# Attention and two expert layers on one core: three tiles' keys and queries fetched as 32x32 squares, one DMA per norm

## The reference, cut to what matters

```python
keep = is_sink | in_window
scores = np.where(keep, scale * q @ k.T, -1e9)
a = np.exp(scores - scores.max(-1, keepdims=True))
attn = (a / (a.sum(-1, keepdims=True) + 1e-9)) @ v      # per batch and head
x = attn.transpose(0, 2, 1, 3).reshape(1536, 512)
x = sum(p[:, e:e+1] * (np.maximum(x @ w1[e], 0) @ w2[e]) for e in range(4))
h = x @ w_in
out = (h * np.cos(h)) @ w_out
```

## Time and profile before

| | us |
|---|---|
| median of 3 runs | 834.82 |
| lowest, highest | 834.08, 837.19 |
| the profiled execution | 837.64 |
| its span | 835.9 |
| TensorE busy in the span | 831.0 (99%) |
| VectorE, ScalarE, GpSimd busy | 455.7, 458.0, 551.7 |
| DMA queue of SyncE | 28.5% of 16 engines |

### The profile page before, as it was taken

The page is one execution under the profiler, slowest core; times in us unless marked ns, Lnnn a source line. Parts: engine busy times, 40 slices in busy tenths (PEclk is TensorE's granted clock), DMA queues, the critical chain, the costliest instruction groups (busy, mean ns, idle before and its releaser), DMA issues.

```text
span 835.9 us, 13778 instructions
## 1 busy us (share of the span) xinstructions
PE 831.0 (99%) x4564; PEld 743.6 (89%) x4564; DVE 455.7 (55%) x947; ACT 458.0 (55%) x985; POOL 551.7 (66%) x417
## 2 busy tenths in 40 slices
PE   9999999999999999999999999999999999999998
PEld 7777989988988988988988998998998998998997
DVE  4988833523523427633433433338767749756756
ACT  5888734334334435433423523525867869867864
POOL 3777996476476778575475575878384399685450
PEclk9999999999999999999999999999999999999999
DMA  8785231211221220432331131130223430530202
GB/s 184 169 190 147 67 123 51 102 61 44 98 68 44 91 83 19 117 105 53 95 112 50 52 101 51 51 101 30 73 63 76 125 117 0 177 102 18 84 1 76
DMA packets 101045, 70.46 MB, mean 84 GB/s; under 512 B 68368, under 2 KB 74864, under 8 KB 100976
## 3 DMA queue, kind: packets, MB, share of 16 engines
q1 hardware_dynamic: 100976, 69.58, 28.5%
HBM read 62.96 MB, written 3.19 MB: 79 GB/s over the span
## 4 chain that ended last, share of the span: by engine, by line
PE 96%; DVE 1%; issue 1%; ACT 1%; DMA 0%; SPq 0%; ACTq 0%; DVEq 0%
PE scores L1499 11%; PE scores L1503 11%; PE scores L1501 11%; PE scores L1512 10%; PE scores L1514 10%; PE scores L1510 10%; PE bank L1512 5%; PE bank L1514 5%; PE bank L1510 5%; PE bank L1499 3%; PE bank L1501 3%; PE bank L1503 3%; PE scores L1406 2%; PE bank L1441 2%; PE bank L1417 1%
## 5 line engine op out<-in xcount | busy, mean ns | idle before, releaser
L665 POOL TENSOR_TENSOR w_lo<-w_raw,w_hi 128x512 fp32r<-128x512 f32 x96 | 129.8, 1362 | 139.0 <-ACT w_hi L814 139.0
L1499 PE MATMUL scores<-x_hi,w_hi 128*128 128x384 f32 x528 | 177.1, 335 | 0.4 <-DVE x_lo L1136 0.2
L1503 PE MATMUL scores<-x_hi,w_lo 128*128 128x384 f32 x528 | 176.8, 335 | 0.0
L1501 PE MATMUL scores<-x_lo,w_hi 128*128 128x384 f32 x528 | 176.5, 334 | 0.0
L672 POOL TENSOR_TENSOR w_lo<-w_raw,w_hi 128x1024 fp32r<-128x1024 f32 x48 | 116.2, 2431 | 65.4 <-ACT w_hi L824 65.4
L824 ACT ACTIVATE w_hi<-w_raw 128x1024 fp32r<-128x1024 f32 x48 | 50.9, 1060 | 190.2 <-PE scores L1514 188.8
L1514 PE MATMUL scores<-w_hi,h_lo 128*128 128x512 f32 x384 | 149.3, 389 | 0.0
L1512 PE MATMUL scores<-w_lo,h_hi 128*128 128x512 f32 x384 | 149.3, 389 | 0.0
L1510 PE MATMUL scores<-w_hi,h_hi 128*128 128x512 f32 x384 | 149.0, 388 | 0.0
L1240 DVE SCALAR_TENSOR_TENSOR acc<-scores,probs,acc 128x512 f32<-128x512 f32 x56 | 41.8, 749 | 116.5 <-PE scores L1514 116.5
L1499 PEld LDWEIGHTS scores<-x_hi,w_hi 128*128 128x128 f32 x528 | 99.1, 188 | 2.4 <-issue 0.7
(11 more groups left out here) (140 smaller groups left out, 1548.0 us busy)
## 6 DMA issues: line engine op xcount, KB each, us to landing
w_raw<-in_moe_w_dram SPq DMA_DIRECT2D x30, 1024.0 KB, 5.1
w_raw<-in_moe_w_in_dram SPq DMA_DIRECT2D x8, 1024.0 KB, 5.0
w_raw<-in_moe_w_out_dram SPq DMA_DIRECT2D x8, 1024.0 KB, 5.4
v_nat<-in_v_dram SPq DMA_DIRECT2D x12, 256.0 KB, 4.0
norm<-routing_dram SPq DMA_DIRECT2D x24, 128.0 KB, 3.2
x_t<-t_sum SPq DMA_DIRECT2D x192, 16.0 KB, 1.9
k_nat<-in_k_dram SPq DMA_DIRECT2D x11, 256.0 KB, 3.8
q_nat<-in_q_dram SPq DMA_DIRECT2D x11, 256.0 KB, 3.6
```

Of the source, the lines that this page charges most:

```text
L665: nc.gpsimd.tensor_tensor(w1_slots(w1_lo, h % 2, part), w1_part(h % 2, part), w1_slots(w1_hi, h % 2, part).bitcast(F32), ALU.subtract)\
L1499: nc.tensor.matmul(target[:, 0:HALF], w1_hi[:, i, slot, d], x_hi[:, n - 1, d], start=first and d == 0, stop=False, skip_group_check=True)
L1501: nc.tensor.matmul(target[:, 0:HALF], w1_hi[:, i, slot, d], x_lo[:, n - 1, d], start=False, stop=False, skip_group_check=True)
L1503: last = nc.tensor.matmul(target[:, 0:HALF], w1_lo[:, i, slot, d], x_hi[:, n - 1, d], start=False, stop=d == 1, skip_group_check=True)
```

## The change

Four things. (1) For the tiles 9, 10 and 11 (SQUARED = 9) there are no loads into `k_nat` and `q_nat` and no transposes by TensorE. 16 DMAs fetch the keys of all three, 16 the queries: each takes one head's 32 columns at 384 positions, 48 KB in pieces of 128 bytes, and places them in 32 partitions, so that a 32x32 transpose of each square by VectorE (`nc.vector.transpose`) gives the tile of `k_t` or `q_t` straight from SBUF. SyncE issues them at the end of its loop's steps t = 2 to 7: 4, 6, 6 for the keys, 6, 6, 4 for the queries. (2) Query copies: tiles 1, 7 and 8 by VectorE, 2 to 6 by ScalarE, 9 to 11 by the new transposes. (3) `load_norm` is one DMA instead of two. The sums stand in another order (even heads first), so that its source is 2 rows of 512 numbers, each read 64 times, and its target 128 partitions of 2 KB. (4) The first two of the first batch's token sums go from VectorE (rounds 18 and 20) to GpSimd (rounds 17 and 19).

```diff
-QUERIES_BY_DVE = (7, 8, 9)
+QUERIES_BY_DVE = (1, 7, 8)
+    SQUARED = T - 3
+    SQUARE_PARTS = 2 * H
+        q_squares = sb("q_squares", [P, PAIRS, HALF], stack=early)
+        k_squares = x_t[:, 1, :, HALF:S]
+        def sum_at(h):
+            return h % 2 * PAIRS + h // 2
...
-            return routing[at:at + rows, :].rearrange("(p r s) e -> p r (s e)", p=PAIRS, r=2)
+            return routing[at:at + rows, :].rearrange("(h s) e -> h (s e)", h=H)
...
+            def load_squares(dst, src, first, last, signal):
+                for n in range(first, last):
+                    h, f = divmod(n, 2)
+                    p, r = divmod(h, 2)
+                    rows = slice((2 * r + f) * 32, (2 * r + f + 1) * 32)
+                    source = src[1, h, (SQUARED - TPB) * P:S, f * 32:(f + 1) * 32]
+                    sp.dma_start(dst[rows, p, :].rearrange("j (c i) -> j c i", i=32),
+                                 source.rearrange("(c j) i -> j c i", j=32)).then_inc(signal, 16)
...
             def load_norm(t):
                 sp.wait_ge(inverse_stored[t % 2], 16 * (t // 2 + 1))
                 if t >= 2:
                     sp.wait_ge(x_ready, t - 1)
-                for r in range(2):
-                    sp.dma_start(norm[r * D:(r + 1) * D, t % 2],
-                                 sums_in_memory(t)[:, r].unsqueeze(0).broadcast_to([D, PAIRS, P]))\
-                        .then_inc(norm_landed[t % 2], 16)
+                sums = sums_in_memory(t).rearrange("(r p) s -> r (p s)", r=2)
+                sp.dma_start(norm[:, t % 2].rearrange("p k s -> p (k s)"),
+                             sums.unsqueeze(1).broadcast_to([2, D, PAIRS * P])).then_inc(norm_landed[t % 2], 16)
...
-                if 5 <= t + 3 < T:
+                if 5 <= t + 3 < SQUARED:
                     load_keys(t + 3)
...
+                if t == 2:
+                    load_squares(k_squares, k, 0, 4, k_squares_landed)
...
+                elif t == 7:
+                    load_squares(q_squares, q, 12, 16, q_squares_landed)
...
@@ GpSimd's rounds
+                if i in (17, 19):
+                    sum_tokens(0, (17, 19).index(i))
@@ VectorE
+                    n = t - SQUARED
+                    nc.vector.transpose(target, k_squares[:, :, n * P:(n + 1) * P]).then_inc(k_ready, 1)
...
+            def turn_queries(t):
+                dve.wait_ge(q_squares_landed, 16 * SQUARE_PARTS)
+                dve.wait_ge(scores_done, PAIRS * (t - 1))
+                n = t - SQUARED
+                nc.vector.transpose(q_t[:, t % 2], q_squares[:, :, n * P:(n + 1) * P]).then_inc(q_squares_ready, 1)
...
-                if i in (18, 20, 21, 23):
-                    sum_tokens((18, 20, 21, 23).index(i))
+                if i == 21:
+                    sum_tokens(2)
+                elif i == 23:
+                    sum_tokens(3)
@@ TensorE's rounds
-                if i % 2 == 1 and (i + 3) // 2 < T:
+                if i % 2 == 1 and (i + 3) // 2 < SQUARED:
                     turn_keys((i + 3) // 2)
-                elif i >= 2 and i % 2 == 0 and i // 2 + 1 < T:
+                elif i >= 2 and i % 2 == 0 and i // 2 + 1 < SQUARED:
                     turn_queries(i // 2 + 1)
```

More of the change, by code:

```diff
@@ L110, in program @@
         x_hi = sb("x_hi", [P, 7, 2, HALF], F32R)
+        early = ExitStack()
+        sb("early_lo", [P, 2, 2, HALF], stack=early)
+        q_squares = sb("q_squares", [P, PAIRS, HALF], stack=early)
+        early.close()
         x_lo = sb("x_lo", [P, 7, 2, HALF], F32R)
@@ L186, in program @@
         first_landed = [sem("first_keys_landed"), sem("first_queries_landed")]
+        k_squares_landed = sem("k_squares_landed")
+        q_squares_landed = sem("q_squares_landed")
         probs_landed = sem("probs_landed")
@@ L204, in program @@
         q_ready = sem("q_ready")
+        q_squares_ready = sem("q_squares_ready")
         k_sink_kept = sem("k_sink_kept")
@@ L427, in store_inverse @@
                 sp.wait_ge(inverse_copied, t + 1)
-                sp.dma_start(sums_in_memory(t).rearrange("p r s -> (p r) s"), inverse[sum_rows(t), t % 2, :])\
+                sp.dma_start(sums_in_memory(t), inverse[sum_rows(t), t % 2, :])\
                     .then_inc(inverse_stored[t % 2], 16)
@@ L518, in _ @@
                     load_values(t)
+                if t == 2:
+                    load_squares(k_squares, k, 0, 4, k_squares_landed)
+                elif t == 3:
+                    load_squares(k_squares, k, 4, 10, k_squares_landed)
+                elif t == 4:
+                    load_squares(k_squares, k, 10, 16, k_squares_landed)
+                elif t == 5:
+                    load_squares(q_squares, q, 0, 6, q_squares_landed)
+                elif t == 6:
+                    load_squares(q_squares, q, 6, 12, q_squares_landed)
+                elif t == 7:
+                    load_squares(q_squares, q, 12, 16, q_squares_landed)
                 if t == TPB + 1:
@@ L647, in normalise @@
                 pool.wait_ge(x_copied, t + 1)
-                pool.wait_ge(norm_landed[t % 2], 32 * (t // 2 + 1))
+                pool.wait_ge(norm_landed[t % 2], 16 * (t // 2 + 1))
                 g, i = divmod(t, TPB)
@@ L780, in exp_head @@
                                      bias=neg_max[:, t, h:h + 1], scale=-1.0,
-                                     accum_out=row_sum[:, t, h:h + 1]).then_inc(exp_ready, 1)
+                                     accum_out=row_sum[:, t, sum_at(h):sum_at(h) + 1]).then_inc(exp_ready, 1)
             def copy_own(d):
@@ L792, in copy_queries @@
                 act.wait_ge(q_turned, t + 1)
[L793 to L796, removed]
+                act.wait_ge(scores_done, PAIRS * (t - 1))
+                nc.scalar.activation(q_t[:, t % 2], turn_bank[:].rearrange("p (k s) -> p k s", k=PAIRS), ACT.Copy)\
                     .then_inc(q_ready, 1)
@@ L916, in _ @@
                     exp_head(i, 1)
-                if i == 1:
-                    copy_queries(1)
                 if 0 <= i - TURN_LAG < ND:
@@ L923, in _ @@
                     exp_head(i, 3)
-                if i >= 2 and i % 2 == 0 and i // 2 + 1 < T and i // 2 + 1 not in QUERIES_BY_DVE:
+                if i >= 2 and i % 2 == 0 and i // 2 + 1 < SQUARED and i // 2 + 1 not in QUERIES_BY_DVE:
                     copy_queries(i // 2 + 1)
@@ L1063, in copy_keys @@
             def copy_keys(t):
-                dve.wait_ge(k_turned, t + 1)
+                if t < SQUARED:
+                    dve.wait_ge(k_turned, t + 1)
+                else:
+                    dve.wait_ge(k_squares_landed, 16 * SQUARE_PARTS)
                 if t >= 3:
@@ L1068, in copy_keys @@
                     dve.wait_ge(k_sink_kept, (t - 3) // TPB + 1)
-                nc.vector.tensor_copy(k_t[:, :, t % 3, 0:P], turn_bank[:].rearrange("p (k s) -> p k s", k=PAIRS))\
-                    .then_inc(k_ready, 1)
+                target = k_t[:, :, t % 3, 0:P]
+                if t < SQUARED:
+                    nc.vector.tensor_copy(target, turn_bank[:].rearrange("p (k s) -> p k s", k=PAIRS))\
+                        .then_inc(k_ready, 1)
+                else:
+                    n = t - SQUARED
+                    nc.vector.transpose(target, k_squares[:, :, n * P:(n + 1) * P]).then_inc(k_ready, 1)
             def copy_queries(t):
                 dve.wait_ge(q_turned, t + 1)
+                if t >= 2:
+                    dve.wait_ge(scores_done, PAIRS * (t - 1))
+                source = out_bank if t == 1 else turn_bank
+                nc.vector.tensor_copy(q_t[:, t % 2], source[:].rearrange("p (k s) -> p k s", k=PAIRS))\
+                    .then_inc(q_ready, 1)
+            def turn_queries(t):
+                dve.wait_ge(q_squares_landed, 16 * SQUARE_PARTS)
                 dve.wait_ge(scores_done, PAIRS * (t - 1))
-                nc.vector.tensor_copy(q_t[:, t % 2], turn_bank[:].rearrange("p (k s) -> p k s", k=PAIRS))\
-                    .then_inc(q_ready, 1)
+                n = t - SQUARED
+                nc.vector.transpose(q_t[:, t % 2], q_squares[:, :, n * P:(n + 1) * P]).then_inc(q_squares_ready, 1)
             def copy_sinks(t):
@@ L1123, in sum_tokens @@
             def sum_tokens(n):
[L1125 to L1128, removed]
+                dve.wait_ge(x_summed, n)
                 nc.vector.tensor_tensor(*token_sum(0, n)).then_inc(x_summed, 1)
@@ L1150, in _ @@
                     copy_keys(1)
+                if i == 1:
+                    copy_queries(1)
                 if i % 2 == 1 and (i + 3) // 2 < T:
                     copy_keys((i + 3) // 2)
-                elif i % 2 == 0 and i // 2 + 1 in QUERIES_BY_DVE:
+                elif i >= 2 and i % 2 == 0 and i // 2 + 1 in QUERIES_BY_DVE:
                     copy_queries(i // 2 + 1)
+                elif i % 2 == 0 and SQUARED <= i // 2 + 1 < T:
+                    turn_queries(i // 2 + 1)
                 if i % 2 == 0 and 0 <= (i - 2) // 2 < T:
@@ L1390, in scores @@
```

(5 more changed lines are left out.)

## The result

The changed kernel takes 859.21 us (median of 5 runs, 858.72 to 860.08), the kernel before 834.82. The ratio is 1.0291, with a 95% interval of 1.0274 to 1.0308. The forecast was 857, slower.

What follows compares the result with a forecast made beforehand. TensorE was taken to set the attention stage's pace; after the change, two DMA engines carrying every norm would, with 70.6 us of work ending the stage 21.7 us later: +22 us, 857 us, likely 850 to 866, wider range 832 to 868.

Steps and rivals of the forecast that it cites:

- Where the norm runs: Norm DMA: with 2 outermost in its source, each norm runs on the same two engines, 128 KB apiece.
- The price of a norm: Norm DMA on two engines: 5.6 us of work taken, bounds 3.8 to 8.9; landing 7.7 us after issue.
- 2.1 + 5.6: Norm's issue to landing: 2.1 us fixed plus 5.6 us for 128 KB on each of two engines.
- The sum: Two engines' work from norm 0 to norm 7: 70.6 us, values of round 23 at 104.5, +22 us overall.
- the terms: Work on the two engines: 5.6 us per norm, 1.12 per 256 KB load, 0.35 per square, 1.4 for w2.
- the two parts of w2 (1.4): DMA engines: two 256 KB parts of the w2 weights, 1.4 us together in the two engines' work.
- GpSimd's sums and VectorE's moves: Sums of 1.85 us each cost nothing to 1.5 us; VectorE's moves, about 0.69 us each, near zero.
- SyncE's queue: SyncE's issuing: squares at 0.6 us each delay norms up to 3 us, costing GpSimd between nothing and 3 us.
- that case: Rival where norms land like before or sooner: 2.6 us saved, 0 to 2.5 taken back, 832 to 835 us.
- the forecast's own case: Attention stage: the norm's two engines become the pace, 857 us, range 850 to 866, chance 0.74.

Runs made afterwards that it cites:

- experiment 1: The changed kernel with the norm in two DMAs again, 64 repeats outermost, pieces still 2 KB: 840.40 us, ratio 1.0053.
- experiment 2: The kernel before with only the norm's single DMA, sums in the new order: 851.81 us, ratio 1.0193.
- experiment 4: The changed kernel with the norm as two DMAs of half the columns, each with 2 rows outermost: 867.78 us, ratio 1.0390.
- experiment 3: The changed kernel with the store of the next tile's sums issued ahead of the norm instead of behind it: 861.12 us, ratio 1.0307.
- experiment 5: The changed kernel with two norm DMAs and the two token sums back on VectorE: 841.32 us, ratio 1.0077.
- experiment 6: The kernel before with only the two token sums moved to GpSimd: 836.15 us, ratio 1.0014.
- experiment 8: The kernel before with only the last three tiles' keys as squares, 16 DMAs spread 3, 3, 3, 3, 4 over steps 2 to 6: 834.29 us, ratio 0.9991.
- experiment 9: The kernel before with only 16 key squares, packed 4, 6, 6 in steps 2 to 4: 840.63 us, ratio 1.0061.
- experiment 7: The kernel before with sums in the new order, its two norm DMAs reading 2 KB pieces: 834.03 us, ratio 0.9990.

## Why the prediction was right, point by point

*Where the norm runs.* Right. That the source's outermost count of 2 puts the norm on two engines was read from a count of packets; experiments 1, 2 and 4 bear it out each in its way, and the signals fit to the unit in the changed kernel and in all three. What the Trainium skill adds ("DMA: Bandwidth & Descriptors", the section on why a DMA increments its semaphore by 16), that it is always the lowest-numbered engines, agrees with experiment 4 as far as that can show it: two DMAs in a row share their pair. Which engines those are no run here shows.

*The price of a norm.* Right. A norm issued at 26.80 was used at 34.59, one issued at 92.67 at 100.69: 7.8 and 8.0 us, where 2.1 + 5.6 were taken. All eight lie between 7.2 and 8.0, 7.7 on the mean.

*The sum.* Right, and by its own terms, for most of the way. The norms of the changed kernel left at 26.80, 37.74, 48.38, 59.64, 68.36, 76.83, 84.84 and 92.67. In steps 3 to 5 (a norm, three loads, six squares) the terms give 5.6 + 3.4 + 2.1 = 11.1 us; the gaps are 10.9, 10.6 and 11.3. In step 6 (one load, six squares) 8.8; it was 8.7. In steps 7 and 9 8.1 each; it was 8.5 and 7.8. In step 8, with a norm and one load, the terms give 6.7, and it was 8.0. There the next norm waited for its sums' store, which landed 7.4 us after its issue, behind the norm before; experiment 3 took that out, and lost as much in other steps. Over the seven steps the terms give 65.0 us and 65.9 were measured.

Part of that agreement is luck. Experiment 2 has no squares: its seven steps took 60.1 us, and less 19 loads of 1.12 and the two parts of w2 (1.4) that leaves 5.3 for a norm, where 5.6 was taken. With 5.3 the seven steps of the changed kernel leave 0.45 us for a square, where 0.35 was taken. These are estimates, in which any pause of the two engines is counted as work. The norms were put too high by 2 us and the squares too low by 3.

The way from there to the end has a second such pair. `normalise` of tile 7 was put at about 102 and came at 100.69, 1.3 us earlier. From it to the values of round 23 the sum had 2.5 us, and it took 4.1: the second cut took 1.35 us instead of 0.63, and the gathering of the sink weights and their turning on TensorE had been left out. So the values began at 104.74, where 104.5 had been worked out. The first product came 21.8 us later than before (105.77 against 83.94 in its profile).

*GpSimd's sums and VectorE's moves.* Right as far as tested. Experiments 5 and 6 show 0.1% either way by their medians for the sums. The new transposes took 0.71 us where 0.69 was taken, and the three of them for keys cost nothing that can be told in experiment 8. The other places of the query copies were not tried alone.

*SyncE's queue.* This is the step that was too small. The forecast said that late norms behind the squares would take back "0 to 2.5" of the 2.6 us saved if the norm was quick, and put that case at 832 to 835 us. Experiment 1 is that case, and it took 840.4. In steps 3 and 4 of the changed kernel six squares took 3.41 us (0.57 each, 0.6 was taken). What I had not counted is that the issues of a step can grow: in experiment 1 those of six squares took up to 4.52 us and that of one tile's values up to 1.87 instead of 0.4. A step of SyncE then lasts 8.3 and 8.5 us (28.38, 36.68, 45.20), longer than a tile of 6.2. From there each late norm is not one delay, covered once by GpSimd's lead, but a new one for every tile in those steps. Experiments 8 and 9 show this for the keys' squares. The last queries' squares also came late: VectorE waited 3.9 us for them in the changed kernel, 2.0 in experiment 1.

This step did not enter the 857, since in the forecast's own case the two engines set the pace. The norm alone costs 16.5 us (experiment 2), the packed squares 5 (experiment 9, and what is left in experiment 1), both together 24.4. How far the 3 us that are left are the squares' work on the two engines was not separated. The sum gave +22, against +21.6 between the two profiled executions; between the medians it was +24.4, because the 2.8 us by which the profiled execution of the kernel before stood above its median had no counterpart in the changed kernel. That is why 857 is 2.2 us low.

## What to carry to other kernels

Read a DMA's outermost count on both sides before merging two into one: a repeat of two rows, each read 64 times, ran on two engines, and the 64-fold repeat outermost on sixteen. In a profile the packets under 512 bytes, less the data pieces, give the signals, and so the engines in use; here the profile of the kernel before was enough to forecast those of the new one. A queue that issues in order has a budget per tile like an engine: add up its issue times for each step, not for the stage, and put new DMAs where a step has room.

## What was not expected of the hardware

The issue of a store or of a tile's values on SyncE took 0.4 to 0.5 us in step 6 of the changed kernel, and 2.6 to 3.1 us in steps 3 to 5, behind a norm on two engines (the store's 2.75 at 38.84 above); six squares then took up to 7.08 us. As I read it, a backlog on two engines holds up the issues for all sixteen. It doesn't take two slow engines to do that: the kernel before had one such issue, that of keys behind eight other DMAs issued since 16.38.

```profile
21.12 4.57 SPq L410 DMA_DIRECT2D k_nat<-in_k_dram  x1
```

TensorE's clock, 1.00 throughout the first 100 us before, was granted at 0.90, 0.84, 0.76 and 0.82 from 20 to 100 us in the changed kernel, a mean of stretches at 2.4 and at 1.2 GHz:

```profile
20.00:40.00 20.00, 16.54 (x161) 12.84 (x159) 14.72 (x66) 13.32 (x51) 9.96 (x19) 0.90 0.68 147
40.00:60.00 20.00, 13.92 (x123) 10.67 (x121) 9.86 (x47) 11.59 (x41) 8.25 (x15) 0.84 0.58 130
60.00:80.00 20.00, 14.31 (x106) 10.31 (x107) 11.39 (x51) 9.08 (x35) 8.96 (x14) 0.76 0.42 95
80.00:100.00 20.00, 17.95 (x148) 12.99 (x148) 12.86 (x58) 12.90 (x46) 13.00 (x20) 0.82 0.40 113
```

It fell after TensorE had waited for GpSimd or for keys, as the 1.97 us at 80.38 behind 4.85 us of idle time show. What the lower clock costs by itself was not measured.

Executions of one kernel also differ by some 3 us in the first 28 us: the first norm left at 28.39 in the profile of the kernel before and at 25.29 in that of experiment 7, whose code up to there differs only in the order of the sums. 2.2 of these 3.1 us are one issue, the keys' at 21.12 above: in experiment 7 it took 2.39 us. Single profiles are therefore no measure of a difference of 3 us here; medians of several runs are.
